# A sparse-attention and two-layer MLP kernel: one load queue reordered, four rounding copies moved from GpSimd to ScalarE, and one copy issued one place later

## The reference: what is computed

```
q, k, v : (4, 8, 576, 64) float32;  tau = 0.02
scores = q @ k^T / sqrt(64)
keep   = scores >= rowmax(scores) - tau          # others get weight 0
attn   = softmax over the kept scores;  a = attn @ v
x  = a as (2304, 512)
h1 = x @ w_in1 (512 x 2048);  g1 = h1 * tanh(softplus(h1));    x2  = g1 @ w_out1
h2 = x2 @ w_in2;              g2 = h2 * clip(h2 + 3, 0, 6) / 6; out = g2 @ w_out2
```

## Time and profile before

| | us |
|---|---|
| median of 3 executions | 1019.16 (1019.05 to 1020.7) |
| the profiled execution: its own time | 1019.16 |
| its span, first to last instruction | 1017.2 |
| PE busy | 996.9 (98%) |
| DVE busy | 867.3 (85%) |
| ACT busy | 626.5 (62%) |
| POOL busy | 504.1 (50%) |

### The profile page before, as it was taken

One profiled execution on the slowest core, in us unless ns is written; L12 is line 12 of the kernel. 1 busy time (PEld: TensorE's weight loads), 2 busy tenths in 40 slices (PEclk: granted clock), 3 DMA queues, 4 the chain that ended last, 5 costly groups with the idle time before them and its releaser, 6 DMA issues.

```text
span 1017.2 us, 20176 instructions
## 1 busy us (share of the span) xinstructions
PE 996.9 (98%) x6984; PEld 932.1 (92%) x6984; DVE 867.3 (85%) x1694; ACT 626.5 (62%) x1145; POOL 504.1 (50%) x512
## 2 busy tenths in 40 slices
PE   5999999999999999999999999999999999999998
PEld 4777778777779999999999999999999999999998
DVE  7999999998966999789997999777996789967884
ACT  5777777778764666466655576456564556645543
POOL 6877678678856810486008820376005740077200
PEclk9999999999999999999999999999999999999999
DMA  6599999899855999499986899444795358753765
GB/s 183 161 249 266 256 251 276 234 267 257 235 170 174 287 319 384 153 286 325 319 303 209 285 304 372 159 151 165 259 312 161 111 199 299 237 161 109 242 240 161
DMA packets 146083, 241.45 MB, mean 237 GB/s; under 512 B 11072, under 2 KB 79168, under 8 KB 145984
## 3 DMA queue, kind: packets, MB, share of 16 engines
q1 hardware_dynamic: 145984, 240.17, 73.6%
HBM read 164.76 MB, written 50.59 MB: 212 GB/s over the span
## 4 chain that ended last, share of the span: by engine, by line
PE 62%; DVE 6%; ACT 5%; issue 3%; DMA 2%; SPq 1%; DVEq 0%; ACTq 0%
PE banks L817 7%; PE banks L818 7%; PE banks L819 7%; PE banks L854 6%; PE banks L853 6%; PE banks L852 6%; PE banks L860 5%; PE banks L861 5%; PE banks L862 5%; ACT relu L1052 3%; PE banks L732 2%; PE banks L673 2%; PE banks L694 2%; DMA ring<-w_out_mix 1%; DVE first_kept L1258 1%
## 5 line engine op out<-in xcount | busy, mean ns | idle before, releaser
L1563 POOL TENSOR_TENSOR ring<-raw,ring 128x256 fp32r<-128x256 f32 x336 | 282.0, 875 | 375.4 <-ACT ring L1017 375.4
L817 PE MATMUL banks<-x_high,ring 128*128 128x384 f32 x672 | 225.8, 336 | 0.6 <-DVE first_kept L1258 0.6
L819 PE MATMUL banks<-x_high,ring 128*128 128x384 f32 x672 | 224.7, 334 | 0.0
L818 PE MATMUL banks<-x_low,ring 128*128 128x384 f32 x672 | 224.6, 334 | 0.0
L854 PE MATMUL banks<-ring,g_low 128*128 128x256 f32 x504 | 142.6, 283 | 0.0
L853 PE MATMUL banks<-ring,g_high 128*128 128x256 f32 x504 | 142.6, 283 | 0.0
L852 PE MATMUL banks<-ring,g_high 128*128 128x256 f32 x504 | 142.6, 283 | 0.0
L950 ACT ACTIVATE exps<-banks,neg_max 128x576 f32<-128x576 f32 x144 | 107.0, 744 | 36.8 <-DVE neg_max L1204 35.9
L817 PEld LDWEIGHTS banks<-x_high,ring 128*128 128x128 f32 x672 | 126.1, 188 | 3.3 <-issue 1.7
L1178 DVE SCALAR_TENSOR_TENSOR probs<-banks,thresh,exps 128x576 f32<-128x576 f32 x144 | 117.2, 814 | 11.2 <-ACT exps L950 4.9
L818 PEld LDWEIGHTS banks<-x_low,ring 128*128 128x128 f32 x672 | 126.2, 188 | 0.0
(11 more groups left out here) (115 smaller groups left out, 2127.0 us busy)
## 6 DMA issues: line engine op xcount, KB each, us to landing
ring<-w_out_mix SPq DMA_DIRECT2D x168, 512.0 KB, 4.9
raw<-w_in_mix SPq DMA_DIRECT2D x48, 896.0 KB, 5.9
w_in_mix<-prep_in SPq DMA_DIRECT2D x18, 896.0 KB, 6.3
w_out_mix<-prep_high SPq DMA_DIRECT2D x16, 896.0 KB, 4.8
w_out_mix<-prep_low SPq DMA_DIRECT2D x16, 896.0 KB, 6.8
prep_in<-w_in SPq DMA_DIRECT2D x64, 128.0 KB, 3.1
prep_out<-w_out SPq DMA_DIRECT2D x64, 128.0 KB, 2.6
k_high<-k_two_high SPq DMA_DIRECT2D x56, 144.0 KB, 3.1
```

The source lines that it names most:

```text
L817: nc.tensor.matmul(dst, w[:, 0, cols], high, start=(t == 0 and m < 4), stop=False, skip_group_check=True)
L818: nc.tensor.matmul(dst, w[:, 0, cols], low, start=False, stop=False, skip_group_check=True)
L819: mm = nc.tensor.matmul(dst, w[:, 1, cols], high, start=False, stop=(t == KH - 1), skip_group_check=True)
L1563: nc.gpsimd.tensor_tensor(ring_slot(slot)[:, 1, :], raw[q % 2][:, m, :], f32(ring_slot(slot)[:, 0, :]), ALU.subtract).then_inc(w_low_ready, 1)
```

## The change

Three edits, and one that follows from the second:

1. SyncE: in iterations 2 to 7, `load_values(it - 1, 1)` moves from before `load_two(it + 1, 0)` and `store_prep_in` to behind both (in iteration 7 there is no `load_two`).
2. GpSimd's `round_x` is gone. ScalarE makes those four x_high tiles, after steps 2, 4, 6 and 8 of the last iteration. The wait for heads 2 and 3 moves with the last two. GpSimd's `rest_x` now stand in one row. The first `round_w` goes from after step 15 to after step 16.
3. In layer 1, `keep_first` of quads 1 to 7 (in round 0 of quads 2 to 7), 20 copies in all, moves behind gate B12 of the quad before. Layer 2 has this order already.

```diff
--- before.py
+++ after.py
@@ -566,11 +566,11 @@
                 if it > 1:
                     load_prep_out(0, it - 1)
                 place_head(it, 1)
-                if it > 1:
-                    load_values(it - 1, 1)
                 if it + 1 < ITS:
                     load_two(it + 1, 0)
                 store_prep_in(0, it - 1)
+                if it > 1:
+                    load_values(it - 1, 1)
                 place_head(it, 2)
             place_head(ITS - 1, 3)
             load_values(ITS - 1, 0)
@@ -999,6 +999,10 @@
                     act.wait_ge(blocks_added, adds_before(r - SPANS + 1, 0))
                     act.wait_ge(c11_kept, r - SPANS + 1)
                 after(act, slot_used, slots_before(r - 1, True))
+                if r == 0 and m in (A12_B21, S4_B22):
+
+                    for k in (2, 3):
+                        act.wait_ge(placed[k], PLACED * (ITS - 1))
                 plain = {A11_B11: B11, A12_B21: B21, S4_B22: B22}
                 src = x_block(r, plain[m]) if m in plain else x_mix[:, m, :, :]
                 nc.scalar.copy(x_high[:, m, :, :], src).then_inc(x_high_ready, 1)
@@ -1073,7 +1077,9 @@
                     attention_step(it, s)
                     if it == ITS - 2 and s in (8, 10, 12):
                         round_x(0, X_ORDER[(8, 10, 12).index(s)])
-                    if it == ITS - 1 and s == 15:
+                    if it == ITS - 1 and s in (2, 4, 6, 8):
+                        round_x(0, X_ORDER[3 + (2, 4, 6, 8).index(s)])
+                    if it == ITS - 1 and s == 16:
                         for k in range(HEADS_IT):
                             act.wait_ge(placed[k], PLACED * (ITS - 1))
                         act.wait_ge(scores_ready, head_used(ITS - 1, 1))
@@ -1100,8 +1106,7 @@
                 for q in range(QUADS):
                     if (r, q) == (0, 0):
                         continue
-                    if q == 0 or (r, q) == (0, 1) or layer_of(r):
-                        keep_first(r, q)
+                    keep_first(r, q)
                     if q + 1 < QUADS:
                         round_w(r, q + 1, 0)
                     else:
@@ -1118,12 +1123,8 @@
                     if unit < LATE_UNITS and part == 1:
                         for n in range(len(LATE_PARTS)):
                             round_prep(*late_unit(unit), n)
-                    for b in (B22, B11):
+                    for b in (B22, B11, B12):
                         gate(r, q, b)
-
-                    if q + 1 < QUADS and not layer_of(r):
-                        keep_first(r, q + 1)
-                    gate(r, q, B12)
                 gate(r, QUADS - 1, B21)
                 for s in range(G_RING, SLOTS):
                     round_g(r, s)
@@ -1533,19 +1534,6 @@
                                (A22_T4, x_block(0, B21), x_mix[:, S2_T2, :, :], ALU.subtract))[n]
                 nc.gpsimd.tensor_tensor(x_mix[:, m, :, :], a, b, op).then_inc(x_mixed, 1)
 
-            def round_x(m):
-
-                if m in X_MIXES:
-                    pool.wait_ge(x_mixed, X_MIXES.index(m) + 1)
-                else:
-
-                    for k in (2, 3):
-                        pool.wait_ge(placed[k], PLACED * (ITS - 1))
-                plain = {A12_B21: B21, S4_B22: B22}
-                src = x_block(0, plain[m]) if m in plain else x_mix[:, m, :, :]
-                ones = one[:, :].to_broadcast([P, KH * WIDE]).rearrange("p (t n) -> p t n", t=KH)
-                nc.gpsimd.tensor_tensor(x_high[:, m, :, :], src, ones, ALU.mult).then_inc(x_high_ready, 1)
-
             def rest_x(m):
 
                 pool.wait_ge(x_high_ready, X_ORDER.index(m) + 1)
@@ -1582,10 +1570,7 @@
                 round_prep(it - 1)
                 rest_prep(it - 1)
 
-
-            for n, m in enumerate(X_ORDER):
-                if n >= 3:
-                    round_x(m)
+            for m in X_ORDER:
                 rest_x(m)
             for quad in range(QUADS * ROUNDS):
                 for m in range(MIXES):
```

## The result

The changed kernel took 1032.5 us (median of 4 runs, 1030.48 to 1037.07) against 1019.11 us for the kernel before on the same chip (4 runs, 1017.17 to 1020.7). The ratio is 1.0139, 95% interval 1.0101 to 1.0177: 13.4 us slower. The forecast was 1028.7 us, so the sign and most of the mechanism were right and the size was too small by 4 us: the prediction had put the clock and edit 3 at nothing, and both cost time. The profiled execution took 1033.37 us, 14.2 us more than the one before; its span is 1031.5 against 1017.2.

The account below looks back on a forecast made before the run. TensorE was taken to set the end, with SP's queue at nearly the same pace in attention. Delay, copies, handover and keep_first: 10.0 + 1.4 - 1.85 + 0 = +9.55 on 1019.16, giving 1028.7 us; 8-in-10 range 1022 to 1032.5.

Parts of the forecast that it names:

- Both hold, the second with 0.2 us to spare: Layer 1, keep_first behind gate B12: TensorE's fifth and sixth products still start on time, so the move costs 0.
- the copies: Last iteration of attention: four x_high copies moved to ScalarE cost 1.4 us in all, bounds 0 and 3.3.
- the landing of the values: Attention, behind the store: values land after TensorE's first use, 3.4 us short in iteration 2, 2.4 in iteration 6.
- gain of 1.85 us at the handover: Attention to layer 1: rounding one step later removes ScalarE's wait for raw weights, -1.85 us, bounds -2.1 and 0.
- The loop's growth: SP's queue, iterations 2 to 6: the loop gets 1.9 us longer each time and adds up; range 1.4 to 2.3.
- rival of a loop that hardly grows: SP's queue: values absorb the hold-up, growth only 0.4 us per iteration, +3.5 us in all, 1022.7 us; chance 0.14.
- TensorE has no idle time with which to catch up: Attention: TensorE can't recover its delays, so its total delay reaches 10.0 us by iteration 6.

Follow-up runs that it names:

- the values ahead of the store: Kernel before, with the value loads moved behind load_two but still ahead of the store: 1029.4 us, ratio 1.0079.
- the five filled waits: Kernel before with edit 1, plus thrown-away identity products on TensorE in five waits for values (18, then 5 each): 1031.08 us, ratio 1.0102.
- the fuller filling: Kernel before with edit 1, plus thrown-away identity products on TensorE in five waits for values (30, then 13 each): 1037.59 us, ratio 1.0156.
- both moves at the handover: Kernel before, with the first raw weights loaded three steps earlier in SP's queue and the first rounding at step 16, not 15: 1019.89 us, ratio 0.9996.

## Why the prediction was right in kind and short in size

In short, four steps failed. The prediction had no term for the clock, which cost 1.7 us. It put edit 3 at 0 ("Both hold, the second with 0.2 us to spare"), which cost 1.4 us in the profile after and 2.7 alone. It had the copies and the landing of the values too small, by 0.9 and 0.8 us. And its gain of 1.85 us at the handover rests on one execution. The rest of this section takes them in turn.

- **The landing of the values** in iteration 2: forecast 88.8 and a wait of 3.4 us, measured 4.4 us and a start at 89.49. The term was 0.7 short, as I read it because I counted the values' 1.4 us of transfer and not their issue: the queue held SP for 1.87 and 1.59 us where the same loads took 1.16 and 0.51 before, and the last load went out at 85.66.
- **The loop's growth**: 1.9 us per iteration forecast and 1.9 measured between these two executions (1.5 over all profiles); TensorE at the mix of iteration 6 is 240.13 - 229.31 = 10.8 us late, forecast 10.0. Of these 10.8 the queue's delay is 7.2 (`load_two` at 231.32 against 224.14), so the landing behind the store falls 3.6 us short of TensorE's need there and not 2.4; in the run with edit 1's order in iteration 6 alone it was 3.85. The rival of a loop that hardly grows is refuted by the single iteration (+4, not +10).
- **The clock**: the missing term. "TensorE has no idle time with which to catch up" was as far as the argument went; that idle time also makes the work behind it slower was not in it. It is 1.7 us after the last wait. The two falls before it don't add to the end in this kernel, since the next wait is shorter by about as much: 0.35 and 0.04 us follow 4.41 and 2.12, and with the clock kept up these two were 1.84 and 2.03. The kernel before gave no warning: its one wait of 2.08 us left the clock at full speed. The Trainium skill tells of it ("TensorE: Matmul & The Clock Gate", HAM oscillation — how this bites in real kernels), for a kernel with DMA waits of about 3 to 5 us: the work behind each wait starts at half clock, every time. This trace agrees for its waits of 2.98 and 4.41 us and shows the same already behind 2.12; other runs show waits of up to 2.39 us without it.
- **The copies on ScalarE**: 1.4 us forecast; the pair that holds them takes 19.98 us and not 17.70, 2.3. The term was mis-sized, within its bounds (0 to 3.3).
- **The handover**: -1.85 forecast, -1.86 between the two profiles. That the numbers agree is luck of the execution that was profiled: the kernel before mostly has no such wait, and no run shows a gain in the time (0.9994 to 0.9998). In the sum below the term stands because the sum is of these two executions; in a forecast of medians it shouldn't.
- **keep_first**: 0 forecast, bound 1 us; both the size and the bound were wrong. Alone it costs 2.7 [1.0, 4.4], and behind the handover the profile after takes 1.4 more, 1.2 of it in single quads. The step that failed is "both hold, the second with 0.2 us to spare". The sixth product was due 0.2 us earlier than I had it, and VectorE, which sets the gate and so the copy, doesn't move in step with TensorE. In the run of edit 3 alone quad 3 starts 0.82 us earlier than before (326.27 against 327.09) and VectorE's chain (328.97 against 329.42) 0.45. A margin of 0.2 us between two engines that aren't locked together is none.

In sum for the profiled executions, in the order growth with landing, clock, copies, handover, keep_first: 10.8 + 1.7 + 2.3 - 1.9 + 1.4 = 14.3 us, against 9.55 forecast; the clock (1.7), keep_first (1.4), the copies (0.9) and the landing (0.8) are the 4.7 us between.

## What to carry to other kernels

Where two chains run at nearly the same pace, ask of a reordered queue not only when its transfers land but how much longer its loop gets, and multiply: one iteration cost 4 us here, five cost 10. Behind a new wait of TensorE of 2 us and more the clock may fall (here it did so behind ten of fourteen); where it does, add 1.7 us, once, for the last such wait on the path. And a spare of a few tenths of a microsecond between engines that no semaphore keeps in step is to be counted as zero. Before a wait in a profile is counted as a gain, look for it in a second profile of the same code; and in a stage where PE is always busy, count the matmuls.

## What the runs showed of the hardware

The fall of the clock needs no DMA. In the run with the raw weights loaded earlier, VectorE's totals of nine elements, 0.16 us at their shortest, lasted 3.85 us. VectorE's timeline there:

```profile
132.73 3.85 DVE L1192 TENSOR_SCALAR totals<-sums 128x9 f32<-128x9 f32 x1
```

GpSimd's at the same time:

```profile
132.54 4.01 POOL L1523 TENSOR_TENSOR prep_low<-prep_out,prep_high 128x1792 fp32r<-128x1792 f32 x1
```

TensorE, which waits for what VectorE does next:

```profile
138.32 0.33 PE L705 MATMUL banks<-ident,recips 128*64 128x64 f32 x4 [2.41 <-DVE x L1185]
```

And the window behind that wait:

```profile
138.90:142.30 3.40, 3.40 (x23) 3.07 (x20) 2.83 (x8) 2.72 (x6) 3.12 (x3) 0.50 1.03 348
```

The tiny operation ends with GpSimd's large one (136.58 and 136.55), TensorE waits 2.41 us for what follows it, and the clock falls for 3.4 us: the pair is 4.0 us longer. Nothing in this stretch differs from the kernel before. It is no single case: of the 224 such totals in all fourteen profiles 126 last over 0.4 us, and each of the 126 ends within 0.1 us of a GpSimd operation that began before it; of the other 98 only one ran while such an operation had more than 0.5 us to go. The Trainium skill says ("SBUF — State Buffer", SBUF: two separate sides) that VectorE and GpSimd share a pair of ports as an exclusive lock, held for the whole instruction, where the VectorE operation is in a two-port mode or has two inputs in SBUF. The common ends agree with a lock; this operation has one input, and no run shows in which mode it was. The kernel before has the same collision up to 2.43 us in its profile, without a fall of the clock behind it. Falls come and go from run to run: of its 29 runs in the last set the 20 with a mean granted clock of 1.000 had a median of 1019.40 us, and the 5 with 0.996 to 0.998 one of 1022.02. That this collision is behind the falls of those runs is not shown.

Between 2 and 2.4 us the length of the wait doesn't decide alone: the clock fell behind waits of 2.02 us (the values ahead of the store, at 87.4) and 2.12, and not behind 2.03 (the five filled waits, at 204.1), 2.08, 2.31 (the fuller filling, at 282.0, again for VectorE) and 2.39. The last is this line of TensorE in the run with both moves at the handover:

```profile
43.88 0.38 PE L673 MATMUL banks<-k_high,q_stack 128*128 128x256 f32 x1 [2.39 <-DMA k_low<-k_two]
```

The granted clock of the 3.4 us behind it is 1.00. The clock fell behind every wait of 2.41 us and more.
